# Zero-tile matmuls at the head of batches 1 to 3 left out, two instead of five to a block in batch 0

## The chip, the cores and the metric

The kernel runs on one core of a Trainium2 chip. The metric is the time of one execution on the device in microseconds (us). Before the change three timed runs gave 1064.76 (median), 1060.64 and 1067.88.

## The reference

There are three stages, on 4 batches of 768 tokens with 8 heads of width 48 (384 channels).

1. A linear recurrence over tokens: for each head a complex 48x48 state is multiplied by a gate row by row and gets the product of key and value added, `S = a*S + k v`, and the output is `y = q S` (real part). The magnitude of a gate is capped at 0.999.
2. Fourier mixing and a channel MLP: `u = y + real(fft over tokens and channels of y)`, layer norm, `relu(un @ w_ch1) @ w_ch2`, and `u` added.
3. A token MLP over the 768 tokens with a residual, then a second channel MLP with a residual.

All of it is float32.

## The kernel before, in words

The recurrence is computed by chunks of 128 tokens: 6 chunks to a batch, 24 in all. One Python loop `for m in range(NM)` on each engine (m is the block, `b, j = divmod(m, 6)`) writes out the order of work. ScalarE (ACT) and VectorE (DVE) prepare the gates of three chunks at a time, in six steps that start six blocks ahead: squares (L690, L691), magnitudes (L696 to L705), inverses and factors (L710 to L719), arctangents (L724 to L728), sines (L735 to L738) on ACT, and between them on DVE the scans (L890, L932) and the products with q and k (L950 to L954). A chunk's q and k are turned by way of DRAM on the DMA queue (L526 to L540).

On TensorE (PE) block m has this order. The keys of chunk m are transposed (L1154; not in the last block of a batch, j = 5). Then the engine waits until DVE has masked the scores of chunk m-1 (L979). Then the outputs of chunk m-1 (L1178 and L1180) and the scores of chunk m (L1162) alternate head by head; the state update follows (L1191; not for j = 5). These are small matmuls, of 48 and 128 columns; in what follows they are called the light work of a block. Behind it, in batch 0, stand the zero-tile matmuls of the change (L1247 by way of L1273); in batches 1 to 3, for j = 1 the middle row and the width transforms of the batch before (L1208, and three groups of 12 instructions at L1223), and for j = 2 to 5 its sequence transforms (L1237 to L1241). Last, the output of chunk m-1 is transposed (L1199), and ACT evacuates that transpose at L758. For j = 0 of batches 1 to 3 (m = 6, 12, 18) there is no Fourier work; behind the transpose stand eight zero-tile matmuls (L1288).

A zero-tile matmul multiplies the identity by a tile of zeros, 128 rows by 384 columns, into a PSUM bank that is cleared by its next user. Its result isn't used. Each one is two matmul instructions in the trace, as every float32 matmul here. Nothing waits for it by a semaphore; but the engine works in order, so that the transpose L1199 in batch 0 and the keys of the next block elsewhere stand behind it.

ACT also works in order. In block m it does, as far as the block has them: arctangents, sines, the copies of the turned keys (L744), squares, magnitudes, inverses and factors, the output of the chunk before (L751), the middle row and the widths (L763, L767), and last the transposed output (L758). So ACT can't begin the arctangents of block m+1 before PE has done the transpose of block m.

The last two stages (the channel and token products, L232 to L242) follow from about 380 us on and are nearly all PE work. The change does not touch them.

Of the kernel before, what the change touches and what calls it, by code (L numbers as in the profile page):

```python
# [13 lines left out]
NT = S // P  # L14
# [283 lines left out]
def forward(nc, ap, lay, c, u_out, x2, out, steep):  # L298
    with ExitStack() as ctx:
# [5 lines left out]
        def sem(name):  # L305
            used.append(nc.alloc_semaphore(name))
            return used[-1]
# [43 lines left out]
        def rounded(name, place, first, *shape):  # L351
            flat = nc.alloc_sbuf_tensor_at(name, [P, math.prod(shape)], fp32r, offset=place + 4 * first)[:, :]
            names = "abcd"[0:len(shape)]
            return flat.rearrange(f"p ({' '.join(names)}) -> p {' '.join(names)}", **dict(zip(names, shape)))

        (w_raw, w_raw_at), (tok_raw, _) = area("w_raw", KD * F), area("tok_raw", NT * DT + KT_ * S)
        (x_flat, _), (w2_flat, w2_flat_at) = area("x_flat", NT * DM), area("w2_flat", KF * DM)
        (w1_area, w1_at), (w2_area, w2_at) = area("w1_area", 2 * KD * F), area("w2_area", 2 * KF * DM)
        (n_area, n_at), (h_area, h_at) = area("n_area", 2 * KD * S), area("h_area", 2 * KF * TG)
# [94 lines left out]
        b_made, b_half, b_added = sem("b_made"), sem("b_half"), sem("b_added")  # L454
# [18 lines left out]
        def transformed_at(j):  # L473
            return {2: [0], 3: [1, 2], 4: [3, 4], 5: [5]}.get(j, [])
# [668 lines left out]
        def _(pe):  # L1143
            mm = nc.tensor.matmul

            def turn_keys(m):
                r = m % RING
                pe.wait_ge(k_back[r], 16 * (m // RING + 1))
                for half in range(2):
                    n = turn_use["k", m, half]  # L1150
                    if n >= 2:
                        pe.wait_ge(tr_free, n - 1)
                    for g in range(4):
                        turned = nc.tensor.transpose(tr_bank[n % 2][:, g * HD2:(g + 1) * HD2], kT[:, r, 4 * half + g, :],  # L1154
                                                     ident[0:HD2, 0:HD2])
                    turned.then_inc(tr_made, 1)

            def score(m, h):
                r = m % RING
                if h % 4 == 0 and m:  # L1160
                    pe.wait_ge(sc_free, 2 * (m - 1) + h // 4 + 1)
                made = mm(sc_bank[h // 4][:, (h % 4) * P:(h % 4 + 1) * P], kT[:, r, h, :], qT[:, r, h, :],  # L1162
                          start=True, stop=True)
                if h % 4 == 3:
                    made.then_inc(sc_made, 1)

            def wait_for_outputs(m):
                pe.wait_ge(sc_free, 2 * (m + 1))
                if m % NCH:
                    pe.wait_ge(st_next, update_no(m - 1) + 1)  # L1170
                if m:
                    pe.wait_ge(y_ready, m)

            def output(m, h):
                p, n = part_of[m], update_no(m) - 1
                cols = slice(h * D, (h + 1) * D)
                later = m % NCH > 0
                made = mm(y_bank[:, cols], pr[:, h, :], v_sb[:, p.s, m - p.first, cols], start=True, stop=not later)  # L1178
                if later:
                    made = mm(y_bank[:, cols], qT[:, m % RING, h, :], state[:, n % 3, cols], start=False, stop=True)  # L1180
                if h == H - 1:
                    made.then_inc(y_made, 1)

            def update(m):
                p, n = part_of[m], update_no(m)
                pe.wait_ge(tr_free, turn_use["k", m, 1] + 1)
                if n:
                    pe.wait_ge(st_free, n)
                for h in range(H):
                    cols = slice(h * D, (h + 1) * D)  # L1190
                    summed = mm(st_bank[0:HD2, cols], kt[:, h, :], v_sb[:, p.s, m - p.first, cols], start=True, stop=True)  # L1191
                summed.then_inc(st_made, 1)

            def turn_y(m):
                n = turn_use["y", m]
                pe.wait_ge(y_ready, m + 1)
                pe.wait_ge(tr_free, n - 1)
                for k_ in range(KD):
                    last = nc.tensor.transpose(tr_bank[n % 2][:, k_ * P:(k_ + 1) * P],  # L1199
                                               y_sb[:, m % YR, k_ * P:(k_ + 1) * P], ident[:, :])  # L1200
                last.then_inc(tr_made, 1)

            def middle(b):
                pe.wait_ge(tr_free, turn_use["y", b * NCH + NCH - 1] + 1)
                if b:
                    pe.wait_ge(b_added, b * NT - 1)
                for k_ in range(KD):
                    last = mm(f_bank[0][0:1, 0:FH], yT[:, k_, S // 2:S // 2 + 1], cd[:, k_, :],  # L1208
                              start=(k_ == 0), stop=(k_ == KD - 1))
                last.then_inc(mid_made, 1)  # L1210

            def width_transform(b, m):
                if m == 0:
                    pe.wait_ge(folded, (b + 1) * KD)
                    if b:
                        pe.wait_ge(b_added, b * NT)
                if m == 1:
                    pe.wait_ge(mid_ready, b + 1)
                if m == 2:
                    pe.wait_ge(a_ready, b * KD + 1)  # L1220
                for part, table in enumerate((cd, sd)):
                    for k_ in range(KD):
                        last = mm(f_bank[(m + 1) % 2][:, part * FH:(part + 1) * FH],  # L1223
                                  fold[:, part, k_, m * P:(m + 1) * P], table[:, k_, :],
                                  start=(k_ == 0), stop=(k_ == KD - 1))
                last.then_inc(a_made, 1)

            def sequence_transform(b, m):
                if m < 2:
                    pe.wait_ge(a_ready, b * KD + 2 + m)  # L1230
                else:
                    pe.wait_ge(b_added, b * NT + m - 1)
                if m == 0:
                    pe.wait_ge(a_ready, (b + 1) * KD)
                rows = slice(m * P, (m + 1) * P)
                out = f_bank[m % 2]
                mm(out[:, 0:FH], alt[:, rows], a_mid[:, :], start=True, stop=False)  # L1237
                for k_ in range(KD):
                    mm(out[:, 0:FH], cs[:, k_, rows], a_sb[:, k_, 0:FH], start=False, stop=(k_ == KD - 1))  # L1239
                for k_ in range(KD):  # L1240
                    last = mm(out[:, FH:2 * FH], ss[:, k_, rows], a_sb[:, k_, FH:2 * FH],  # L1241
                              start=(k_ == 0), stop=(k_ == KD - 1))
                last.then_inc(b_made, 1)

            def keep_busy(count):
                for _ in range(count):
                    mm(f_bank[0][:, 0:S // 2], ident[:, :], blank[:, :], start=True, stop=True)  # L1247
# [6 lines left out]
            for m in range(NM):  # L1254
                p, r = part_of[m], m % RING
                b, j = divmod(m, NCH)
                if j < NCH - 1:
                    turn_keys(m)
                if m:
                    wait_for_outputs(m - 1)  # L1260
                    for h in range(ahead):
                        output(m - 1, h)
                pe.wait_ge(k_back[r], 16 * (m // RING + 1))
                pe.wait_ge(q_back[r], 16 * (m // RING + 1))
                for h in range(H):
                    score(m, h)
                    if m and h + ahead < H:
                        output(m - 1, h + ahead)
                pe.wait_ge(v_in[p.s], 16 * (p.turn + 1))
                if j < NCH - 1:  # L1270
                    update(m)
                if m < NCH:
                    keep_busy(5)  # L1273
                if m == NCH:
                    pe.wait_ge(wide_tables_in, 5 * 16)
                if b and j == 1:
                    middle(b - 1)
                    for n in range(KD):
                        width_transform(b - 1, n)
                if b:  # L1280
                    for n in transformed_at(j):
                        sequence_transform(b - 1, n)
                if m:
                    turn_y(m - 1)
                if b and j == 0:
                    if b > 1:
                        pe.wait_ge(b_added, (b - 1) * NT - 1)
                    keep_busy(8)  # L1288
            wait_for_outputs(NM - 1)
            for h in range(H):  # L1290
                output(NM - 1, h)
# [736 lines left out]
```

## Time and profile before

| | |
|---|---|
| timed runs, us | 1060.64, 1064.76 (median), 1067.88 |
| profiled execution, us | 1054.72 |
| its span, first to last instruction, us | 1052.7 |
| mean granted TensorE clock | 0.982 |
| recurrence and Fourier stage ends at about, us | 380 |

The profiled execution's own time is 2.0 us more than its span, and 10.0 us less than the median of the timed runs. Times in the rows below count from the first instruction. A granted clock of 1.00 is 2.4 GHz and 0.50 is 1.2 GHz.

### The profile page before, as it was taken

To read this page: it belongs to the slowest core of one execution; us is meant where nothing else is said; L and a number is where in the kernel's file an instruction comes from. 1 tells how busy PE (TensorE), PEld (TensorE's weight loads), DVE (VectorE), ACT (ScalarE), POOL (GpSimd) and SP (SyncE) were. 2 spreads that over 40 slices of the span, in tenths; PEclk is the share of its full clock that TensorE was granted. 3 is DMA by queue.
4 is the path that set the end of the run, shared out by engine and by line. 5 is a ranking of instruction groups with operands and counts; after the bars stand their busy time and mean duration, and the time that the engine had idled before them with its cause. 6 is when DMAs were issued, how large, how long until landed. Compare 5 with 4: busy or idle time off the path is not lost.

```text
span 1052.7 us, 15640 instructions
## 1 busy us (share of the span) xinstructions
PE 987.1 (94%) x6154; PEld 947.3 (90%) x6154; DVE 514.6 (49%) x980; ACT 357.9 (34%) x532; POOL 16.4 (2%) x12
## 2 busy tenths in 40 slices
PE   0389999999999999999999999999999999999997
PEld 0268889889899899999999999999999999999997
DVE  5888799999946654324234322542323314223220
ACT  7676666676621510220220221431203102121220
POOL 0000000000000000000000000030000000000000
PEclk9789899999999999999999999999999999999999
DMA  6689977986785056021021020010001001000000
GB/s 207 196 233 246 263 227 185 228 260 145 187 238 205 16 192 221 16 75 45 15 75 45 22 68 23 16 53 16 8 24 45 22 15 52 22 0 22 9 16 25
DMA packets 96602, 104.68 MB, mean 99 GB/s; under 512 B 13089, under 2 KB 90145, under 8 KB 96546
## 3 DMA queue, kind: packets, MB, share of 16 engines
q1 hardware_dynamic: 96546, 103.94, 33.8%
q8 instruction: 35, 0.57, 0.2%
q14 instruction: 21, 0.17, 0.1%
HBM read 70.80 MB, written 33.11 MB: 99 GB/s over the span
## 4 chain that ended last, share of the span: by engine, by line
PE 77%; DVE 12%; ACT 7%; issue 2%; DMA 0%; SPq 0%; DVEq 0%; ACTq 0%
PE bank L232 21%; PE bank L233 21%; PE bank L234 21%; DVE n_area L932 3%; PE bank L1162 2%; PE bank L1223 2%; PE bank L1180 2%; PE bank L1239 2%; PE bank L242 1%; PE bank L1178 1%; PE bank L1241 1%; DVE n_area L937 1%; PE bank L1191 1%; PE bank L1247 1%; DVE n_area L920 1%
## 5 line engine op out<-in xcount | busy, mean ns | idle before, releaser
L120 ACT ACTIVATE hh<-bank 128x384 fp32r<-128x384 f32 x192 | 94.5, 492 | 377.1 <-PE bank L234 377.1
L208 DVE SCALAR_TENSOR_TENSOR hl<-bank,hh 128x384 fp32r<-128x384 f32 x192 | 107.1, 558 | 195.5 <-ACT hh L120 195.5
L232 PE MATMUL bank<-w2h,hh 128*128 128x384 f32 x576 | 193.2, 335 | 0.0
L232 PE MATMUL bank<-nTh,w1h 128*128 128x384 f32 x576 | 193.0, 335 | 0.0
L234 PE MATMUL bank<-w2h,hl 128*128 128x384 f32 x576 | 192.5, 334 | 0.0
L234 PE MATMUL bank<-nTh,w1l 128*128 128x384 f32 x576 | 192.5, 334 | 0.0
L233 PE MATMUL bank<-nTl,w1h 128*128 128x384 f32 x576 | 192.4, 334 | 0.0
L233 PE MATMUL bank<-w2l,hh 128*128 128x384 f32 x576 | 192.4, 334 | 0.0
L232 PEld LDWEIGHTS bank<-nTh,w1h 128*128 128x128 f32 x576 | 108.1, 188 | 0.4 <-issue 0.3
L233 PEld LDWEIGHTS bank<-w2l,hh 128*128 128x128 f32 x576 | 108.2, 188 | 0.0
L232 PEld LDWEIGHTS bank<-w2h,hh 128*128 128x128 f32 x576 | 108.1, 188 | 0.0
L233 PEld LDWEIGHTS bank<-nTl,w1h 128*128 128x128 f32 x576 | 108.1, 188 | 0.0
L234 PEld LDWEIGHTS bank<-nTh,w1l 128*128 128x128 f32 x576 | 108.1, 188 | 0.0
L234 PEld LDWEIGHTS bank<-w2h,hl 128*128 128x128 f32 x576 | 108.1, 188 | 0.0
L1162 PE MATMUL bank<-w_area 96*128 96x128 f32 x384 | 76.0, 304 | 0.3 <-DMA w_area<-q_turn 0.3
L222 DVE TENSOR_TENSOR late_area<-bank,tok_raw 128x384 f32<-128x384 f32 x24 | 13.4, 558 | 125.1 <-PE bank L234 125.1
L1247 PE MATMUL bank<-late_area,ident 128*128 128x384 f32 x120 | 46.9, 545 | 28.5 <-DVE w_flat L951 28.5
L1178 PE MATMUL bank<-w_area 128*128 128x48 f32 x384 | 65.0, 254 | 2.4 <-DVE w_area L979 2.4
L1247 PEld LDWEIGHTS bank<-late_area,ident 128*128 128x128 f32 x120 | 25.0, 216 | 44.9 <-issue 34.1
L1180 PE MATMUL bank<-late_area,w_area 96*128 96x48 f32 x320 | 62.6, 278 | 0.0
L113 ACT ACTIVATE nTh<-bank 128x384 fp32r<-128x384 f32 x48 | 22.3, 490 | 113.6 <-PE bank L242 113.3
L1178 PEld LDWEIGHTS bank<-w_area 128*128 128x128 f32 x384 | 58.1, 193 | 3.1 <-DVE w_area L979 3.1
(153 smaller groups left out, 1292.4 us busy)
## 6 DMA issues: line engine op xcount, KB each, us to landing
w_area<-k_turn SPq DMA_DIRECT2D x24, 384.0 KB, 4.6
w_area<-q_turn SPq DMA_DIRECT2D x24, 384.0 KB, 6.0
q_turn<-w_raw SPq DMA_DIRECT2D x30, 192.0 KB, 2.8
k_turn<-n_area SPq DMA_DIRECT2D x24, 192.0 KB, 2.5
k_turn<-w_flat SPq DMA_DIRECT2D x24, 192.0 KB, 2.7
u_scratch<-h_area SPq DMA_DIRECT2D x24, 192.0 KB, 6.4
w_raw<-in_moe_w_ch SPq DMA_DIRECT2D x2, 2304.0 KB, 13.0
x_flat<-u_scratch SPq DMA_DIRECT2D x4, 1152.0 KB, 10.3
```

The source lines that it names most:

```text
L113: self.nc.scalar.activation(self.nTh[:, :, i * P:(i + 1) * P], self.tr_bank[i % 2][:, 0:DM].rearrange("p (k t) -> p k t", k=KD), ACT.Copy) ...
L120: self.nc.scalar.activation(self.hh[:, m, :], self.mm_bank[(g * (KF + TPG) + m) % 2][:, 0:TG], ACT.Relu).then_inc(self.h_high, 1)
L208: self.nc.vector.scalar_tensor_tensor(out=self.hl[:, m, :], in0=self.mm_bank[(g * (KF + TPG) + m) % 2][:, 0:TG], scalar=0.0, in1=self.hh[: ...
L232: self.nc.tensor.matmul(out, lh, rh, start=(n == 0), stop=False)
L233: self.nc.tensor.matmul(out, lh, rl, start=False, stop=False)
L234: last = self.nc.tensor.matmul(out, ll, rh, start=False, stop=(n == len(pairs) - 1))
L932: last = V.tensor_tensor_scan(t3_b[s][:, g, T], t3_b[s][:, g, T], t4[:, g, offset], start, ALU.add, ALU.add)
L1162: made = mm(sc_bank[h // 4][:, (h % 4) * P:(h % 4 + 1) * P], kT[:, r, h, :], qT[:, r, h, :], start=True, stop=True)
L1178: made = mm(y_bank[:, cols], pr[:, h, :], v_sb[:, p.s, m - p.first, cols], start=True, stop=not later)
L1180: made = mm(y_bank[:, cols], qT[:, m % RING, h, :], state[:, n % 3, cols], start=False, stop=True)
L1223: last = mm(f_bank[(m + 1) % 2][:, part * FH:(part + 1) * FH], fold[:, part, k_, m * P:(m + 1) * P], table[:, k_, :], start=(k_ == 0), sto ...
L1247: mm(f_bank[0][:, 0:S // 2], ident[:, :], blank[:, :], start=True, stop=True)
```

## The change

The eight zero-tile matmuls of m = 6, 12 and 18 are left out, with a wait for DVE in front of them for m = 12 and 18. In the six blocks of batch 0 there are two instead of five. The six at the start (L1252) stay. In all, 60 zero-tile matmuls become 18.

```
                 if m < NCH:
-                    keep_busy(5)
+                    keep_busy(2)
...
                 if m:
                     turn_y(m - 1)
-                if b and j == 0:
-                    if b > 1:
-                        pe.wait_ge(b_added, (b - 1) * NT - 1)
-                    keep_busy(8)
```

## Rows read from the trace of the kernel before

**Rows 1.** The page: busy time; the chain by engine; the zero-tile group (count, busy us, mean ns, idle before).
```profile
PE 987.1 (94%) x6154; PEld 947.3 (90%) x6154; DVE 514.6 (49%) x980; ACT 357.9 (34%) x532; POOL 16.4 (2%) x12
...
PE 77%; DVE 12%; ACT 7%; issue 2%; DMA 0%; SPq 0%; DVEq 0%; ACTq 0%
...
L1247 PE MATMUL bank<-late_area,ident 128*128 128x384 f32 x120 | 46.9, 545 | 28.5 <-DVE w_flat L951 28.5
```

**Rows 2.** The chain that ended last, blocks 2 to 5: start us, us, what.
```profile
82.22 3.29 PE bank L1247 x10
...
85.88 0.49 ACT w_area L758
86.37 1.05 ACT n_area L724
...
98.76 0.69 DVE w_area L979
...
109.78 4.87 PE bank L1247 x10
...
120.34 3.23 PE bank L1247 x10
```

**Rows 3.** Timeline of PE in batch 0: start us, us, engine, line [idle before].
```profile
58.43 5.05 PE L1247 MATMUL bank<-late_area,ident 128*128 128x384 f32 x10
...
64.85 0.87 PE L1178 MATMUL bank<-w_area 128*128 128x48 f32 x6 [0.71 <-DVE w_area L979]
...
69.84 3.46 PE L1247 MATMUL bank<-late_area,ident 128*128 128x384 f32 x10
73.84 0.55 PE L1199 MATMUL bank<-ident,h_area 128*128 128x128 f32 x3 [0.54 <-ACT h_area L751]
...
75.35 0.35 PE L1178 MATMUL bank<-w_area 128*128 128x48 f32 x2
...
80.74 1.48 PE L1191 MATMUL bank<-w_area 128*96 128x48 f32 x16
82.06 3.46 PE L1247 MATMUL bank<-late_area,ident 128*128 128x384 f32 x10
...
99.50 0.42 PE L1178 MATMUL bank<-w_area 128*128 128x48 f32 x2 [1.07 <-DVE w_area L979]
...
107.10 2.69 PE L1191 MATMUL bank<-w_area 128*96 128x48 f32 x16
109.58 5.07 PE L1247 MATMUL bank<-late_area,ident 128*128 128x384 f32 x10
114.50 0.49 PE L1199 MATMUL bank<-ident,h_area 128*128 128x128 f32 x3
```

**Rows 4.** Timeline of PE, blocks 6 and 7, then the start of block 19.
```profile
131.92 5.33 PE L1247 MATMUL bank<-late_area,ident 128*128 128x384 f32 x16
...
137.09 0.82 PE L1154 MATMUL bank<-ident,w_area 96*128 96x96 f32 x8
137.75 0.85 PE L1178 MATMUL bank<-w_area 128*128 128x48 f32 x6
...
142.82 1.14 PE L1208 MATMUL bank<-res_area,w_area 128*1 128x193 f32 x6
143.89 2.23 PE L1223 MATMUL bank<-res_area,w_area 128*128 128x193 f32 x12
146.93 4.20 PE L1223 MATMUL bank<-res_area,w_area 128*128 128x193 f32 x24 [0.80 <-ACT late_area L763]
...
286.68 0.87 PE L1178 MATMUL bank<-w_area 128*128 128x48 f32 x6 [0.44 <-DVE w_area L979]
```

**Rows 5.** Windows: stretch, busy of PE, PEld, DVE, ACT, POOL; granted clock; DMA share; GB/s.
```profile
40.00:42.00 2.00, 0.00 (x0) 0.00 (x0) 1.05 (x2) 2.00 (x2) 0.00 (x0) 0.79 0.69 199
60.00:62.00 2.00, 2.00 (x5) 1.04 (x4) 1.90 (x6) 0.00 (x0) 0.00 (x0) 0.59 0.89 226
102.00:104.00 2.00, 2.00 (x15) 2.00 (x14) 1.97 (x3) 1.97 (x3) 0.00 (x0) 0.65 0.66 71
112.00:114.00 2.00, 2.00 (x6) 1.05 (x5) 1.97 (x7) 0.00 (x0) 0.00 (x0) 0.79 0.88 256
134.00:136.00 2.00, 2.00 (x8) 1.18 (x7) 1.93 (x5) 0.00 (x0) 0.00 (x0) 1.00 1.06 395
```

## The prediction

> **What bounds the kernel now.** I read the page first. PE is busy for 94% of the span and holds 77% of the chain that ended last; the zero-tile matmuls are 120 instructions that keep it busy for 46.9 us [rows 1]. That looks like work to save. But the change touches only the first third of the span, where DVE and ACT hold long stretches of the chain, so I asked next for the chain in order of time. Of the six zero-tile blocks of batch 0 three stand on it, those of blocks 2, 4 and 5 (3.29, 4.87 and 3.23 us), and none of the three heads m = 6, 12, 18 [rows 2]. The reader is to see how they get on it: ACT does the transposed output of the block (L758) before the next arctangents (L724), and that transpose stands behind the zero tiles on PE. From there the chain goes by ACT and DVE to the mask (L979) at 98.76, for which PE waits.
>
> The timeline of PE shows the other side. Block 0's zero tiles are followed by a wait for the mask, block 1's by a wait for ACT, and block 3's by the 1.07 us wait for the mask before 99.50 [rows 3]. At the heads the tiles run from 131.92 to 137.09, the keys take until about 137.75, and there the mask arrives: PE goes on at once [rows 4]. In block 19 the outputs wait for the mask until 286.68. So the head's eight tiles fill a wait and cost about 0.15 us.
>
> Last I read the granted clock in windows. It is at half speed (1.2 GHz) in two stretches of this part: from about 41 to 61.6 us and from about 102.6 to 112.8 us. In the first, PE had no work when it began; the second began 3 us after an idle gap of only 1.07 us with light work behind it [rows 3, 5]. In the second all of the light work of block 4 from 102.6 on ran at half speed and didn't bring the clock back. Both times it came back during the zero tiles (they began at 58.43 and 109.58, about 3.2 us before) [rows 3, 5]. During the head's tiles, from 134 to 136, it is at 1.00 [rows 5].
>
> **The change part by part.** One zero tile is two instructions. At full clock ten take 3.29 us, so 0.33 us each [rows 2]; at half clock 0.66.
>
> Block 2: six instructions less is 1.97 us on the chain. ACT and DVE could take the next step that much earlier: L758 had waited for PE. -1.97.
>
> Block 5: the same, -1.97.
>
> Block 3: nothing of the tiles; the wait for the mask covers them. But the idle gap grows from 1.07 to 3.0 us, so I take block 4 at half clock from its start. The light work of a block with an update takes 82.06 - 75.35 = 6.7 us at full clock. At half clock the update's row goes from 82.06 - 80.74 = 1.32 to 109.58 - 107.10 = 2.48 us, a factor of 1.88 [rows 3]. So block 4 takes 12.6 instead of 109.58 - 99.50 = 10.1 us: +2.5. Its four zero-tile instructions at half clock take 2.6 instead of 4.87 us: -2.3. Together +0.2.
>
> Block 0 and 1: after the first block's tiles PE idles 0.71 us; without six of ten instructions it idles some 3 us, less if the clock stays low longer. The nearest gap (1.07 us) brought the clock down. Block 1's light work, 69.84 - 64.85 = 5.0 us, then takes 9.4, until 74.25; with 2.6 us of tiles its transpose comes at 76.9 instead of 73.84: +3.1 [rows 3].
>
> Batch 0 sums to +3.1 - 1.97 + 0.2 - 1.97 = -0.6 us. Its bounds: all at full clock, which is the second rival below (-10.8), and blocks 2 and 5 at half clock too, the third (+13).
>
> The heads: 16 instructions less each. Their cover is the wait for the mask, so taking them out gains 0.15 us at most. What they leave is an idle gap from about 132.7 (the keys, 0.8 us, move up to 131.92) to 137.7, 5.0 us. The gap that was followed by half clock in block 4 was a fifth of this. So I take block 7's light work at half clock. It takes 142.82 - 137.75 = 5.07 us now; by 1.88 it takes 9.5, +4.5. L1208 (1.07 us) adds 1.07. The clock came back about 3.2 us after dense matmuls began both times; L1208 and the first 1.1 us of L1223 are that, so L1223 adds 0.55. Less the 0.15 the head gains, 6.0 us. Against that stands the 0.80 us by which the next L1223 waits for ACT today [rows 4]: 5.2 us. That row is on the chain from there: L1223, the light work of block 8, and then L758 and L724. It repeats at block 13 with the same 0.80. At block 19 there is no such wait: 6.1. The three heads are 5.2 + 5.2 + 6.1 = +16.5 us. The bounds for one head: the clock returns in the middle of the light work (about 2.3 - 0.8 = +1.4, or 2.3 for block 19), or all twelve L1223 instructions run at half clock too (+1.7 more).
>
> The waits left out with them (for DVE's additions before block 12 and 18) cost nothing: L1208 has the same wait in the block behind. No DMA is moved; transfers for later chunks only get more time.
>
> Sum: 16.5 - 0.6 = +15.9 us. Against the profiled execution (1052.7 span and 2.0 around it, 1054.7) that is 1070.6. The timed runs lie 10.0 us above it in the median; the profile doesn't show why, so I keep the difference and add the sum to the median: 1064.8 + 15.9 = **1080.7 us**.
>
> **The rivals.** What this kernel's runs can tell from no change is about 1%, 10.6 us; the three runs themselves spread over 7.2.
>
> *First rival, the clock costs little.* It returns in the middle of each light block: 1.4 + 1.4 + 2.3 - 0.6 = +4.5, 1069 us. For it: half-clock work in block 4 was a little denser than the same work at full clock, since all of it is slower. Against it: seven microseconds of that work, 102.6 to 109.58, didn't bring it back [rows 3, 5]. The Trainium skill (TensorE: Matmul & The Clock Gate, Part 1, "What's actually happening") says that for modelling, the ramp penalty is under 1% of a typical kernel's span; by that rule the sum would be at most 10.5 us, so no more than about 1075. The trace's mean clock of 0.982 doesn't test it, since for most of its low time PE was idle.
>
> *Second rival, faster.* One mechanism: the clock stays up in batch 0 and the zero tiles were plain cost on the chain. Then block 4's 10.08 + 4.87 = 14.95 us [rows 2, 3] become 6.7 + 1.3 = 8.0, -6.9; with blocks 2 and 5 that is -10.8, and the heads give 0: 1054 us; if block 4 keeps its low stretch, 1057 to 1059. It decides at the idle gap before each mask: if PE can stand idle for 3 to 5 us at full clock, this is the outcome. Against it: PE stood idle when the clock fell at 41 us, and a gap of 1.07 us was enough before 102.6 [rows 3, 5].
>
> *Third rival, batch 0 goes low altogether.* Two tiles don't bring the clock back where five did. Block 2 then takes 12.6 + 2.6 instead of 6.7 + 1.3 (+7.2), block 5, whose light work takes 120.34 - 114.50 - 0.4 = 5.4 us, 10.2 + 2.6 instead of 5.4 + 1.3 (+6.1): 13 us more than forecast, 1094. For it: at half clock two tiles last 2.6 us, less than the 3.2 us after which the clock came back both times. Against it: the light work beside them counts for something.
>
> **How the numbers follow.** Forecast (1073 to 1088) 0.55; first rival (1065 to 1075) 0.17; second rival 0.12, half of it over 1% faster when all of batch 0 stays up; third 0.16. Faster by over 1%: 0.05. Within 1%: the rest of the second rival (0.07), the first (0.17) and the low edge of the forecast (0.03), 0.27. Slower by over 1%: 0.68. The range leaves out the second rival and the upper part of the third: 1064 to 1092.
>
> **What would show it.** In the profile after, the granted clock should be 0.50 behind each of 132, 206 and 280 us (shifted), through the light work of blocks 7, 13 and 19, and back at 1.00 within L1223; L1178 to L1191 there should take about 9.5 us instead of 5.1. The first L1223 group should be followed by no wait for ACT. The chain should lose L1247 in blocks 2 and 5 by 2 us each. The mean clock should fall below 0.982 by about three times 13 us at half, to some 0.965. The forecast is wrong if the clock is at 1.00 in block 7, or if it returns before L1208.

## The result and the profile after

| | before | after |
|---|---|---|
| median, us | 1062.7 (4 runs, 1057.38 to 1067.88) | 1083.28 (4 runs, 1076.04 to 1086.02) |
| profiled execution, us | 1054.72 | 1076.04 |
| span, us | 1052.7 | 1074.0 |
| mean granted clock | 0.982 | 0.948 |

The ratio is 1.0204, with a 95% interval of 1.0157 to 1.025, against 1080.7 us forecast: the kernel got slower, by about 2%. The forecast held in sign and, for the heads, in mechanism. The medians are 20.6 us apart, where its sum was 15.9; it did not see one thing that both kernels do, and which is told below.

The page of the changed kernel, rows as in [rows 1]:

```profile
PE 992.2 (92%) x6070; PEld 960.5 (89%) x6070; DVE 514.6 (48%) x980; ACT 358.5 (33%) x532; POOL 16.4 (2%) x12
...
PE 80%; DVE 12%; ACT 4%; issue 2%; DMA 0%; SPq 0%; DVEq 0%
...
L1247 PE MATMUL bank<-late_area,ident 128*128 128x384 f32 x36 | 20.2, 713 | 28.3 <-DVE w_flat L951 28.3
```

The zero tiles fell from 46.9 to 20.2 us of busy time, and yet PE is busy for 5 us more. Work that the change doesn't touch takes longer. Where, the timeline of PE at the first head shows (start us, us, engine, line [idle before]); it answers to [rows 4]:

```profile
130.72 0.51 PE L1199 MATMUL bank<-ident,h_area 128*128 128x128 f32 x3
...
136.95 1.52 PE L1178 MATMUL bank<-w_area 128*128 128x48 f32 x6 [4.58 <-DVE w_area L979]
...
143.94 2.69 PE L1191 MATMUL bank<-w_area 128*96 128x48 f32 x16
146.55 2.09 PE L1208 MATMUL bank<-res_area,w_area 128*1 128x193 f32 x6
148.57 6.97 PE L1223 MATMUL bank<-res_area,w_area 128*128 128x193 f32 x36
155.38 0.49 PE L1199 MATMUL bank<-ident,h_area 128*128 128x128 f32 x3
```

The mask arrives where it did before, 0.8 us earlier because batch 0 ended so much earlier. PE has waited 4.58 us for it, and the light work of block 7 takes 146.55 - 136.95 = 9.6 us instead of 5.07. The 36 instructions of L1223 now run without the wait of 0.80 us for ACT. The third head (block 19) is the same: 5.13 us idle, then 9.6 us.

```profile
295.70 1.52 PE L1178 MATMUL bank<-w_area 128*128 128x48 f32 x6 [5.13 <-DVE w_area L979]
...
302.69 2.69 PE L1191 MATMUL bank<-w_area 128*96 128x48 f32 x16
305.31 2.08 PE L1208 MATMUL bank<-res_area,w_area 128*1 128x193 f32 x6
```

The windows of the changed kernel (stretch, busy time of PE, PEld, DVE, ACT, POOL, granted clock, DMA share, GB/s) show the clock falling within each gap and returning inside the Fourier matmuls, or at the third head just before them (at about 307.2 us; L1223 starts at 307.32). They answer to [rows 5]:

```profile
136.00:138.00 2.00, 1.05 (x5) 1.06 (x6) 2.00 (x3) 2.00 (x3) 0.00 (x0) 0.65 0.67 207
150.00:152.00 2.00, 2.00 (x13) 2.00 (x13) 2.00 (x8) 0.36 (x1) 0.00 (x0) 0.94 1.04 269
214.00:216.00 2.00, 0.00 (x0) 0.00 (x0) 1.90 (x6) 0.82 (x1) 0.00 (x0) 0.77 0.95 339
228.00:230.00 2.00, 2.00 (x10) 1.78 (x10) 2.00 (x5) 0.32 (x1) 0.00 (x0) 0.81 1.03 289
292.00:294.00 2.00, 0.00 (x0) 0.00 (x0) 1.93 (x5) 0.00 (x0) 0.00 (x0) 0.90 0.62 125
306.00:308.00 2.00, 2.00 (x9) 0.97 (x8) 1.97 (x4) 0.32 (x1) 0.00 (x0) 0.69 0.99 270
```

In batch 0 the timeline (it answers to [rows 3]) shows both gaps grown, from 0.71 to 2.65 us before block 1 and from 1.07 to 2.98 us before block 4, each followed by light work at half clock:

```profile
64.70 1.36 PE L1178 MATMUL bank<-w_area 128*128 128x48 f32 x6 [2.65 <-DVE w_area L979]
...
76.71 0.85 PE L1199 MATMUL bank<-ident,h_area 128*128 128x128 f32 x3
...
100.90 0.42 PE L1178 MATMUL bank<-w_area 128*128 128x48 f32 x2 [2.98 <-DVE w_area L979]
...
112.40 2.89 PE L1247 MATMUL bank<-late_area,ident 128*128 128x384 f32 x4
```

One more low stretch stands where the change does nothing. In block 20 light work runs at full clock until 317.5, and then at half, though the last wait of PE was one of 0.31 us, 3.0 us earlier:

```profile
314.45 0.55 PE L1154 MATMUL bank<-ident,w_area 96*128 96x96 f32 x4 [0.31 <-ACT w_area L758]
...
317.10 0.32 PE L1178 MATMUL bank<-w_area 128*128 128x48 f32 x2
318.02 0.50 PE L1178 MATMUL bank<-w_area 128*128 128x48 f32 x2
...
322.72 2.69 PE L1191 MATMUL bank<-w_area 128*96 128x48 f32 x16
```

The starts of the transposes (L1199) at the end of each block give the balance. Each number is after less before, in us, in the two profiled executions:

| block | 1 | 2 | 3 | 4 | 5, 6 | 7 to 12 | 13 to 18 | 19 | 20 | 21 on |
|---|---|---|---|---|---|---|---|---|---|---|
| late by | +2.87 | +1.41 | -0.52 | +0.59 | -0.85 | +4.41 | +9.03 | +14.48 | +20.55 | +20.91 |

So batch 0 gives -0.85, the three heads +5.26, +4.62 and +5.45 (together +15.3), and the stretch in block 20 (it reaches into block 21) +6.4. The stages from there add nothing but 0.4 us.

### The profile page after: what moved, and what is told of

The parts are those of the page before. It is cut to its first block, busy times and chain, and to the rows that moved or that the text cites. A ratio compares the mean times of both kernels' runs of the same rounds, so it can differ in the third digit from the quotient of the medians.

```text
span 1074.0 us, 15472 instructions
## 1 busy us (share of the span) xinstructions
PE 992.2 (92%) x6070; PEld 960.5 (89%) x6070; DVE 514.6 (48%) x980; ACT 358.5 (33%) x532; POOL 16.4 (2%) x12
## 4 chain that ended last, share of the span: by engine, by line
PE 80%; DVE 12%; ACT 4%; issue 2%; DMA 0%; SPq 0%; DVEq 0%
PE bank L232 20%; PE bank L233 20%; PE bank L234 20%; PE bank L1162 4%; DVE n_area L932 3%; PE bank L1223 2%; PE bank L1178 2%; PE bank L1191 2%; PE bank L1180 2%; PE bank L1239 2%; PE bank L242 1%; PE bank L1241 1%; DVE n_area L937 1%; DVE n_area L920 1%; DVE w_area L979 1%
## 5 line engine op out<-in xcount | busy, mean ns | idle before, releaser
L1178 PE MATMUL bank<-w_area 128*128 128x48 f32 x384 | 72.2, 277 | 20.2 <-DVE w_area L979 20.2
L1162 PE MATMUL bank<-w_area 96*128 96x128 f32 x384 | 87.6, 339 | 0.4 <-DMA w_area<-q_turn 0.4
L1178 PEld LDWEIGHTS bank<-w_area 128*128 128x128 f32 x384 | 66.9, 220 | 21.1 <-DVE w_area L979 21.1
L222 DVE TENSOR_TENSOR late_area<-bank,tok_raw 128x384 f32<-128x384 f32 x24 | 13.4, 557 | 125.1 <-PE bank L234 125.1
L1162 PEld LDWEIGHTS bank<-w_area 96*128 96x128 f32 x384 | 64.5, 225 | 0.5 <-issue 0.5
L222 DVE TENSOR_TENSOR late_area<-bank,res_area 128x384 f32<-128x384 f32 x24 | 13.4, 556 | 92.6 <-PE bank L234 92.6
```

The source lines that it names most:

```text
L222: self.nc.vector.tensor_tensor(self.out_sb[:, i % 2, :], self.mm_bank[2 + t % 2][:, 0:DM], self.res[:, i, :], ALU.add).then_inc(self.out_r ...
```

## The experiments

The main theory: with the heads' tiles out, PE idles for 5 us, the clock falls, and the light work behind runs at half speed. The rivals: batch 0 pays, or the clock has no part in it. Each experiment was timed beside runs of the kernel before; differences in us are of medians, and where the text says "in the profile" they are of the starts of the L1199 transposes (L1201 with two lines added above) in two profiled executions.

**1. The two halves of the change alone.** First only the heads:

```
-                if b and j == 0:
-                    if b > 1:
-                        pe.wait_ge(b_added, (b - 1) * NT - 1)
-                    keep_busy(8)
```

> Only the heads' eight zero tiles are left out; batch 0 keeps five to a block. My theory (the clock falls in the idle gap and the light work of blocks 7, 13 and 19 runs at half speed): +15 us (the three heads gave +5.3, +4.6 and +5.5 in the profile of the changed kernel), a ratio of 1.012 to 1.017, and half clock from the gap to L1223 in each. Rival (batch 0's missing tiles cost it): no change, 1.000.

Measured: 1081.65 us against 1057.6, ratio 1.0218 (1.0149 to 1.0287). Then only batch 0:

```
-                    keep_busy(5)
+                    keep_busy(2)
```

> Only batch 0 is changed, two tiles to a block; the heads keep their eight. My theory: -0.6 us by the forecast's sum, with runs that go low more often in batch 0 (up to +6), so a ratio of 0.997 to 1.004; the heads stay at full clock. Rival (batch 0 pays the whole loss): 1.015 to 1.02.

Measured: 1058.59 against 1057.6, ratio 1.0005 (0.9944 to 1.0067). The loss comes with the heads; batch 0 is nothing within the noise, as forecast. But the first ratio is more than the heads' 15.3 us allow: they make 1.0145, just outside its interval. The profiled execution of the first kernel, the slowest of its four runs (1090.55), tells more. Its heads cost 4.7, 4.4 and 5.3 us, and besides them it went to half clock three more times in the light work of batches 1 to 3, each time for about 6.4 us of delay. The timeline of one of them, with columns as above:

```profile
268.16 0.55 PE L1154 MATMUL bank<-ident,w_area 96*128 96x96 f32 x4 [0.25 <-ACT w_area L758]
...
270.51 0.45 PE L1162 MATMUL bank<-w_area 96*128 96x128 f32 x2
...
271.18 0.75 PE L1162 MATMUL bank<-w_area 96*128 96x128 f32 x2
```

The kernel with only batch 0 changed had two such stretches too (it fell at 228.8 and 259.5 us), with its heads at full clock. I call them chance stretches: the profiled execution of the kernel before has none between 113 and 355 us, and the same instructions run at full clock in other batches. They have one thing in common. Nine of them stand in the profiles of the changed kernel and of experiments 1 to 4 (the transforms moved, below, not counted), and each began 3.0 to 3.1 us after the wait of 0.25 to 0.31 us between the two halves of the key transposes (268.16 and 271.2 here; 314.45 and 317.5 in the changed kernel). The runs of before fit this. In the largest set, 19 runs, those at 1054 to 1057 us have a mean clock of 0.981 or 0.982, those at 1060 to 1065 us of 0.973 to 0.975, and two at 1065.7 and 1066.1 of 0.969. That is nearly the step of one stretch. One such stretch would be the larger part of the 10 us between profile and median that the forecast left unexplained; those runs have no profile, so this is inferred. It is also open whether leaving out the heads' tiles makes such stretches more frequent: these four runs and those of the changed kernel exceed what the heads cost, but they are few.

**2. Does the gap's length matter?** Four tiles instead of eight at the heads:

```
-                    keep_busy(8)
+                    keep_busy(4)
```

> Four instead of eight zero tiles at the heads; batch 0 as before. PE idles some 2.4 us before the mask instead of 0 or 5. Theory A (any idle gap of that size brings the clock down, as 1.07 us did in block 4): nearly the same loss as with none, +12 to +22 us, 1.012 to 1.02. Theory B (the loss goes with the length of the gap): about half, 1.006 to 1.01.

Measured: 1080.25 against 1062.99, ratio 1.0151 (1.0066 to 1.0237). The interval also takes in most of theory B's range, so it is the profile that decides for theory A. The timeline of its first head:

```profile
131.93 2.75 PE L1247 MATMUL bank<-late_area,ident 128*128 128x384 f32 x8
...
137.73 0.87 PE L1178 MATMUL bank<-w_area 128*128 128x48 f32 x6 [2.39 <-DVE w_area L979]
...
142.56 2.69 PE L1191 MATMUL bank<-w_area 128*96 128x48 f32 x16
145.18 2.09 PE L1208 MATMUL bank<-res_area,w_area 128*1 128x193 f32 x6
```

About half the gap (2.39, 2.74 and 3.00 us) was still followed by half clock at each of the three heads. In the profile they cost 3.8, 5.0 and 4.8 us, 13.6 together, against 15.3 with no tiles: the first rows at 137.73 ran at full speed, because here the clock fell 2.4 us after the gap. Half the tiles buy back a ninth of the loss.

**3. Is it enough to be busy?** At the heads 32 tiles of 48 columns in place of eight of 384:

```
+            def keep_lightly_busy(count):
+                for _ in range(count):
+                    mm(f_bank[0][:, 0:D], ident[:, :], blank[:, 0:D], start=True, stop=True)
...
-                    keep_busy(8)
+                    keep_lightly_busy(32)
```

> Batch 0 as before; at the heads, in place of eight zero tiles of 384 columns, 32 of 48 columns, the size of the output matmuls: PE is about as long busy with an eighth part of the columns of each. Theory A (an idle engine brings the clock down): full clock in blocks 7, 13 and 19, a ratio of 1.000. Theory B (what counts is how many columns stream, not whether the engine has an instruction): the clock falls at the heads as with none, +10 to +15 us, 1.010 to 1.015.

Measured: 1090.21 against 1057.6, ratio 1.0293 (1.023 to 1.0356), worse than with no tiles (1081.65 in the same set). The timeline and the windows of the first head:

```profile
133.83 9.79 PE L1251 MATMUL bank<-late_area,ident 128*128 128x48 f32 x64
143.42 1.51 PE L1154 MATMUL bank<-ident,w_area 96*128 96x96 f32 x8
144.72 1.41 PE L1178 MATMUL bank<-w_area 128*128 128x48 f32 x6
```

```profile
136.00:138.00 2.00, 2.00 (x20) 2.00 (x20) 1.93 (x5) 0.00 (x0) 0.00 (x0) 1.00 1.07 380
138.00:140.00 2.00, 2.00 (x12) 2.00 (x12) 1.97 (x5) 1.78 (x2) 0.00 (x0) 0.54 1.01 341
150.00:152.00 2.00, 2.00 (x12) 2.00 (x12) 0.85 (x2) 1.70 (x3) 0.00 (x0) 0.50 1.04 287
```

The engine is busy for 2.00 of 2.00 us in every window, and the clock falls at 138 all the same. It fell inside the filler at the second head too, at 223.5; before the third it had already fallen in the light work of block 18, at 298.6. Then the filler itself runs at half speed, outlasts the mask (block 7 goes on at 144.72; the kernel before, 1.9 us ahead at that point, at 137.75), and the light work behind is at half speed as well. In the profile the heads cost 10.5, 10.2 and 15.5 us. The overrun, 5.1 of the 10.5 us at the first, was not priced by theory B; it is why the loss is twice what it gave. So theory A is out: the clock fell without an idle gap. What it is in the small tiles that lets it fall is not separated here: they have fewer columns each, and PE loads weights all the time with them (PEld 2.00 of 2.00 us, against 1.18 in the window 134:136 of [rows 5]).

**4. Can it be turned round?** If gaps before the mask bring the clock down, filling those of batch 0 and cutting only where tiles stand on the chain should gain:

```
-                    keep_busy(5)
+                    keep_busy((6, 5, 2, 7, 2, 2)[m])
```

> The heads keep eight; the six blocks of batch 0 have 6, 5, 2, 7, 2 and 2 zero tiles, so that those before a wait for the mask (blocks 0 and 3) fill it, and those on the chain (2, 4, 5) are cut. My theory: block 4 stays at full clock, -10 us against before, a ratio of 0.990. Rival (the clock falls in block 4 whatever fills the gap): -4 us, 0.996.

Measured: 1064.27 against 1057.6, ratio 1.0049 (1.0002 to 1.0096): no gain. The profile shows that half the theory held. Block 4 ran at full clock, as it did in all four profiles with this filling. (With the gap of about 1.05 us left open it fell to half clock in six profiles of eight.) Its transpose started 6.9 us earlier than before (107.64), where it had to wait 1.64 us for ACT:

```profile
103.16 1.48 PE L1191 MATMUL bank<-w_area 128*96 128x48 f32 x16
104.48 1.52 PE L1247 MATMUL bank<-late_area,ident 128*128 128x384 f32 x4
107.64 0.55 PE L1199 MATMUL bank<-ident,h_area 128*128 128x128 f32 x3 [1.64 <-ACT h_area L751]
```

But the clock fell one block later, at 108.6, which cost 3.7 of the 6.9 us back, and in blocks 9 and 20 there were chance stretches of 6.4 us each. So the next question was what brings those. The candidate is the wait of 0.25 us for ACT between the two halves of the key transposes, with only light work on both sides, 3 us after which each of them began. It can be filled at no cost, with a zero tile into the bank of outputs, which is free at that point:

```
                 for half in range(2):
                     n = turn_use["k", m, half]
                     if n >= 2:
+                        if half:
+                            mm(y_bank[:, 0:144], ident[:, :], blank[:, 0:144], start=True, stop=True)
                         pe.wait_ge(tr_free, n - 1)
```

> As the kernel before, and in each block with keys one zero tile of 144 columns more, between the two halves of the key transposes, where PE waits 0.25 us for ACT. Theory (the extra low stretches of 6.4 us, which in some runs stand in light blocks of batches 1 to 3, come from light work together with that wait): these stretches go away, the tile fits the wait, and the time falls to that of the fastest runs of before, -3 to -6 us in the median (0.995 to 0.997), with less spread. Rival (they come by chance whatever is done): +0 to +2 us for the tiles, 1.000 to 1.002.

Measured: 1053.74 against 1062.99, ratio 0.990 (0.9819 to 0.9981). Its timeline shows that the tile fits where the wait was (the second half of the keys starts 0.75 us after the first; in the kernel before 0.74, from 123.74 to 124.48), and its windows that no low stretch is left between 100 and 346 us:

```profile
118.90 0.50 PE L1156 MATMUL bank<-ident,w_area 96*128 96x96 f32 x4
119.24 0.44 PE L1153 MATMUL bank<-late_area,ident 128*128 128x144 f32 x2
119.65 0.55 PE L1156 MATMUL bank<-ident,w_area 96*128 96x96 f32 x4
```

```profile
150.00:200.00 50.00, 50.00 (x404) 47.25 (x403) 46.08 (x89) 35.41 (x41) 0.00 (x0) 1.00 0.84 216
200.00:250.00 50.00, 49.09 (x369) 44.03 (x369) 45.72 (x91) 32.12 (x42) 0.00 (x0) 1.00 0.79 202
250.00:300.00 50.00, 49.82 (x377) 45.18 (x376) 42.40 (x83) 26.27 (x35) 0.00 (x0) 1.00 0.72 190
```

That includes block 4: though PE idled 1.04 us before it as ever, the clock stayed up, and all of the 4.8 us by which this execution is ahead of the profiled one of before at the end of batch 3 come from there. So the gain of the medians is not that of the chance stretches alone.

```profile
99.58 0.42 PE L1180 MATMUL bank<-w_area 128*128 128x48 f32 x2 [1.04 <-DVE w_area L979]
```

A repeat in more rounds measured less:

> The tile of 144 columns in the key wait alone, once more on the same chip: 0.990 of before; if the cut of batch 0's tiles is worth anything beside it, this kernel is slower than the one with the cut by 1 to 4 us.

Measured: 1055.14 (12 runs) against 1058.25, ratio 0.9953 (0.9925 to 0.998). It had no chance stretch in batches 1 to 3 in its profile either, but block 4 was at half clock again, and that alone put it 6.6 us behind the other. The gain is real in both sets, 0.5 to 1.0% by the medians.

With the tile and the counts 6, 5, 2, 7, 2, 2 together:

> The tile of 144 columns in the key wait, and in batch 0 the counts 6, 5, 2, 7, 2 and 2 of the kernel that filled the gaps. Theory: block 4 at full clock and no chance stretches, -10 us against before, 0.990. Rival (with two tiles to a block the clock falls somewhere in batch 0 or 1 all the same): 0.997 to 1.003.

Measured: 1049.66 against 1062.99, ratio 0.9849 (0.9776 to 0.9922), the theory or better. And once more in more rounds:

> The best kernel so far once more, in more rounds: the tile of 144 columns in the key wait, and 6, 5, 2, 7, 2 and 2 zero tiles in batch 0. If its time of 1049.7 us in four runs was the rule: 0.984 to 0.99 of before and a spread of a few us. If it was luck (chance stretches as in the kernel with five tiles in block 4): 0.990 to 0.995.

Measured: 1050.61 (6 runs, 1048.85 to 1052.51) against 1058.25, ratio 0.992 (0.9891 to 0.9949). By the ratio this is the case that was called luck; but the kernel's own time is 1 us from the first set's, and it is the runs of before that were 4.7 us faster here. On the same chip the kernel with the tile alone took 1055.14, so the counts are worth about 4.5 us beside it. This is the best version: 8 to 13 us faster than the kernel before, some 33 faster than the changed one by the medians (on other chips), and with a spread of 1.1 us in four runs and 3.7 in six, where the runs of before, of which there were more, spread over 13. In the profile of the first set the clock falls once between 61 and 350 us, in block 5:

```profile
61.00:108.00 47.00, 44.70 (x332) 37.54 (x332) 43.05 (x72) 35.62 (x41) 0.00 (x0) 1.00 0.87 242
108.00:120.00 12.00, 12.00 (x58) 11.02 (x57) 9.62 (x21) 6.92 (x7) 0.00 (x0) 0.57 1.03 319
120.00:350.00 230.00, 226.11 (x1737) 206.35 (x1735) 188.33 (x380) 125.83 (x164) 1.33 (x1) 1.00 0.74 203
```

Two tries to go on failed. Five tiles in block 4, to save block 5:

```
-                    keep_busy((6, 5, 2, 7, 2, 2)[m])
+                    keep_busy((6, 5, 2, 7, 5, 2)[m])
```

> As the kernel with the tile in the key wait and 6, 5, 2, 7, 2, 2 in batch 0, but with five instead of two tiles in block 4, behind which its clock fell at 109 us. Theory: block 5 stays at full clock, which is worth 3.0 us against 2.0 for the tiles, so 0 to -2 us against that kernel (0.983 to 0.985 of before). Rival (it falls at another place): 0.985 to 0.99.

Measured: 1054.83 against 1061.48, ratio 0.9939 (0.991 to 0.9967), beyond even the rival's range. Block 5 did run at full clock, and its transpose started 8.7 us earlier than before. But then PE was so far ahead that it stood idle for 2.96 us until the DMA had brought the keys of block 6. The clock fell in that gap, at 117.8, and the whole light work of block 6 ran at half clock:

```profile
118.20 0.90 PE L1156 MATMUL bank<-ident,w_area 96*128 96x96 f32 x4 [2.96 <-DMA w_area<-k_turn]
```

```profile
117.00:136.00 19.00, 17.80 (x83) 16.77 (x84) 15.78 (x30) 9.16 (x11) 0.00 (x0) 0.55 0.87 204
```

And the sequence transforms moved into the middle of the light work:

```
                     if m and h + ahead < H:
                         output(m - 1, h + ahead)
+                    if b and h == H // 2 - 1:
+                        for n in transformed_at(j):
+                            sequence_transform(b - 1, n)
...
-                if b:
-                    for n in transformed_at(j):
-                        sequence_transform(b - 1, n)
```

> As the kernel before, but the sequence transforms of a block (dense matmuls of 193 columns) stand in the middle of its light work instead of behind it. Theory (long light work is what brings the chance stretches): the stretches go away, -3 to -6 us in the median, unless a transform has to wait for DVE there, which costs up to 1 us a block. Rival (no effect on the clock): 1.000 or slower.

Measured: 1081.93 against 1062.99, ratio 1.014 (1.0061 to 1.022). The gain did not come and the cost was mis-sized: a transform had to wait for DVE for up to 2.77 us, not 1. The clock fell at 200.0, 1 us after this gap, and six times in all in batches 1 to 3.

```profile
199.00 0.59 PE L1237 MATMUL bank<-late_area,tok_raw 1*128 1x193 f32 x2 [2.77 <-DVE h_area L1005]
```

So whether long light work alone brings chance stretches was not tested by it, because the move added gaps of its own.

**5. The heads with chance out of the way.** The tile in the key wait, and the heads' eight tiles out, batch 0 as before (the two edits shown above together):

> The tile of 144 columns in the key wait, batch 0 as before (five to a block), no zero tiles at the heads: against the kernel with that tile and with the heads' eight this is the heads alone, with the chance stretches out of the way. Theory: three falls, +15 to +16.5 us against that kernel (0.990), so 1.004 to 1.007 against the kernel before. Rival (the chance stretches come back because the heads start them): 1.012 or more.

Measured: 1067.13 against 1061.48, ratio 1.0087 (1.0053 to 1.0122), between the theory and the rival. Against the first set of the kernel with the tile and with the heads' tiles the medians are 13.4 us apart, on different chips. In the profile, which has no chance stretch, the heads cost 4.4, 5.9 and 6.0 us, 16.3 together; 16.5 was the forecast. The clock outside the heads, in the windows between them, is 1.00:

```profile
64.00:130.00 66.00, 62.88 (x481) 54.15 (x479) 58.42 (x99) 49.62 (x58) 0.00 (x0) 1.00 0.87 244
130.00:146.00 16.00, 12.99 (x62) 11.48 (x63) 15.68 (x28) 10.62 (x12) 0.00 (x0) 0.57 0.94 256
146.00:208.00 62.00, 60.91 (x486) 57.42 (x484) 53.45 (x107) 41.07 (x50) 0.00 (x0) 1.00 0.83 203
208.00:228.00 20.00, 16.13 (x72) 14.61 (x73) 19.55 (x39) 11.12 (x13) 0.00 (x0) 0.57 0.85 260
```

Its ten runs fall in two groups, six at 1065.8 to 1067.4 and four at 1072.2 to 1074.2, so some runs still have a low stretch more. It can be a chance stretch or block 4 at half clock, as in the repeat above; the times do not tell the two apart. The kernel with the tile and the heads' tiles has such groups too: its lower one, two runs at 1050.2 and 1050.25, is 16 us below the lower one here.

## Why the prediction was right

**The heads.** Forecast 5.2 + 5.2 + 6.1 = 16.5 us. The changed kernel's profile has 5.26, 4.62 and 5.45, 15.3 together; with chance stretches out of the way it is 16.3. Its terms held: idle 4.58 to 5.13 us (forecast 5.0), light work 9.6 us (9.5), L1208 2.1 us (2.14), and the wait of 0.80 for ACT gone. Only the last part, 0.55 us of L1223 at half clock, varied: at the third head the clock was back before L1223 began, and this head cost 5.45 instead of 6.1. That the loss comes with the heads and not with batch 0 is shown by the two halves run alone.

**Batch 0.** Forecast -0.6, in the profile -0.85, in the runs +1.0 within noise. Block 1 lost 2.87 (3.1 forecast). The chain lost 1.9 us of L1247 in each of blocks 2 and 5, as forecast, but their transposes gained only 1.46 and 1.44 us instead of 1.97, because the clock came back only at 78.5 and 116.1 and their first rows ran at half speed. Block 4 gained 0.81 from the mask on where a loss of 0.2 was forecast, because its first 1.6 us still ran at full clock.

**The rivals.** The first, that the clock returns within the light work, is refuted by all profiles with a gap at a head. With it goes the reading of the Trainium skill's sentence (TensorE: Matmul & The Clock Gate, "What's actually happening") that the ramp penalty is under 1% of a typical span: here the heads alone cost 15.3 of 1052.7 us, 1.5%, since a kernel that falls and returns at every stage pays each time. The summary table of the same page of the Trainium skill ("Why this matters for your kernels") advises against idle gaps between bursts of matmuls. The traces agree: all gaps before the masks of the heads, from 2.39 to 5.13 us, went with a fall. Shorter ones with light work behind were followed by a fall at times: one of about 1.05 us before block 4 in six profiles of eight, and the wait of 0.25 to 0.31 us nine times. So the forecast's reading of the 1.07 us gap, "enough", was right for most executions and not for all. The second rival, full clock in batch 0 as plain gain, did not come about with two tiles to a block. Its sum of -10.8 was also too large: with the gap filled the kernel was 6.9 us ahead after block 4, where ACT became the wait, and at most 8.7 after block 5, where the DMA of the keys did. The third did not come: the clock was back within 2 us after the two tiles of blocks 1 and 4.

**What failed.** "I keep the difference and add the sum to the median" stood on an open difference of 10.0 us between the profile and the runs. The forecast's sum has no term for a fall in light work without a gap, and the changed kernel's profile has one, +6.4 us. In differences it shows: the sum was 15.9 us, the medians are 20.6 apart and the profiled executions 21.3, so what is missing is about one such stretch. The total came within 2.6 us partly by luck, because a fourth run of the kernel before (1057.38) lowered its median from 1064.8 to 1062.7. The mean clock was forecast at about 0.965 and came out at 0.948: the estimate counted the three heads alone. Between 62 and 350 us the profile has six low stretches of some 13.7 us: the heads, block 1, block 4 (10.2 us there before) and block 20.

## What to carry to other kernels

A matmul that computes nothing can be worth more than it costs. Before taking one out, look at what it stands in front of: if PE waits there anyway it costs nothing, and then the question is at what clock the next light work runs; if it stands on the chain of waits, it costs its time. Fill waits to the full with wide tiles, since half a filling or narrow tiles saved little or did harm here. Look for short waits in the middle of long light work, where one small tile gained 0.5 to 1%. And find out what the engine will wait for next once it runs ahead: here it was first ACT and then the DMA of the keys, and the clock fell in or right behind the new gap.

## What the runs showed of the hardware that was not expected

- PE busy without a break, but with matmuls of 48 columns, did not hold the clock: it was 1.00 from 136 to 138 us and 0.54 in the mean from 138 to 140, with 2.00 of 2.00 us busy in both, and it fell at the second head in the same way.
- The clock fell in light work 3.0 to 3.1 us after a wait of 0.25 to 0.31 us, nine times, in some executions and some blocks only. Where it was measured alone it lost the kernel about 6.4 us. Why one block and not the next is not settled; the profiles show the same instructions in both.
- None of the six profiled executions with a tile of 144 columns in that wait has such a stretch; of the eight without it five have (and the one with the transforms moved has falls of its own). Whether the tile works by filling the wait or by its columns was not separated, and the runs of three of these kernels still fall in groups some 5 to 7 us apart.
